# A long fused kernel on one core: x loaded once a batch and turned by VectorE instead of TensorE

## What is computed

```python
# 1: batch 4, heads 8, seq 768, head_dim 48
for t in range(S):
    state = alpha[:, :, t, :, None] * state + einsum('bhd,bhe->bhde', k[:, :, t], v[:, :, t])
    y[:, :, t] = einsum('bhd,bhde->bhe', q[:, :, t], state)
# 2: x is y with the heads side by side, (4, 768, 384)
theta = x @ w_theta
zr, zi = x * cos(theta), x * sin(theta)
y = einsum('ts,bsd->btd', w_tok_r, zr) + einsum('ts,bsd->btd', w_tok_i, zi)
u = x + y
x = u + maximum(u @ w_ch, 0)
# 3: d_ff 1024
h = maximum(x @ w_in, 0)
conv = sum over k of conv_w[k] * (h shifted by k - 1 tokens)
out = (h * sigmoid(conv)) @ w_out
```

## Time and profile before

| | us |
|---|---|
| three runs | 531.9, 532.3, 532.47 |
| median | 532.3 |
| span of the profiled execution, first to last instruction | 530.5 |
| TensorE busy in it | 522.1 |
| VectorE busy | 441.2 |
| ScalarE busy | 287.4 |

### The profile page before, as it was taken

How to read it: one execution, slowest core, us unless ns; L and a number is a source line. 1 busy time by engine, 2 the same in 40 slices (tenths; PEclk the granted TensorE clock), 3 DMA queues, 4 the chain that set the end, 5 groups by cost and what they waited for, 6 DMA issues and landing times.

```text
span 530.5 us, 11806 instructions
## 1 busy us (share of the span) xinstructions
PE 522.1 (98%) x4142; PEld 513.2 (97%) x4142; DVE 441.2 (83%) x801; ACT 287.4 (54%) x607; POOL 72.0 (14%) x65
## 2 busy tenths in 40 slices
PE   8999999999999999999999999999999999999997
PEld 7999988999999999999999999999999999999997
DVE  8999996997886759767786777999888888889874
ACT  4889887765534434444344542555555454545353
POOL 5988893000000000000000000000000000000000
PEclk9999999999999999999999999999999999999999
DMA  8999987476131020211062011202020110201011
GB/s 326 336 308 361 313 302 224 120 236 222 40 104 31 17 70 25 96 30 54 15 205 94 1 45 56 80 2 90 0 89 30 59 56 33 89 0 47 0 46 44
DMA packets 37163, 56.93 MB, mean 107 GB/s; under 512 B 3328, under 2 KB 27392, under 8 KB 37120
## 3 DMA queue, kind: packets, MB, share of 16 engines
q1 hardware_dynamic: 34000, 51.65, 29.3%
q10 hardware_dynamic: 3120, 4.72, 2.5%
HBM read 42.20 MB, written 14.16 MB: 106 GB/s over the span
## 4 chain that ended last, share of the span: by engine, by line
PE 92%; SPq 2%; DVE 2%; DMA 2%; issue 1%; ACT 0%; POOL 0%; DVEq 0%; ACTq 0%
PE y_bank L1475 26%; PE y_bank L1534 19%; PE theta_bank L1521 10%; PE x_bank L1521 10%; PE y_bank L1505 7%; PE theta_bank L1462 7%; PE weighed L1372 4%; PE x_sum L1330 3%; PE x_sum L1345 2%; PE turned L1357 2%; SPq L734 1%; PE x_bank L1450 1%; DMA x_in<-x_scratch 1%; PE turned L1377 1%; PE x_sum L1316 1%
## 5 line engine op out<-in xcount | busy, mean ns | idle before, releaser
L1534 PE MATMUL y_bank<-first_w,z 128*128 128x384 f32 x576 | 109.5, 335 | 0.0
L1534 PEld LDWEIGHTS y_bank<-first_w,z 128*128 128x128 f32 x576 | 101.2, 188 | 0.0
L1475 PE MATMUL y_bank<-first_w,z 128*128 128x384 f32 x432 | 78.0, 337 | 0.1
L1475 PE MATMUL y_bank<-rest_w,z 128*128 128x384 f32 x432 | 76.9, 336 | 0.0
L1475 PEld LDWEIGHTS y_bank<-first_w,z 128*128 128x128 f32 x432 | 74.5, 188 | 0.3 <-issue 0.3
L1475 PEld LDWEIGHTS y_bank<-rest_w,z 128*128 128x128 f32 x432 | 74.7, 188 | 0.0
L1045 ACT ACTIVATE out_rows<-theta_bank 128x386 f32<-128x386 f32 x32 | 15.8, 493 | 50.6 <-PE theta_bank L1521 50.5
L1275 DVE TENSOR_SCALAR x_rows<-out_rows,taps 128x384 f32<-128x384 f32 x64 | 26.8, 419 | 19.5 <-ACT out_rows L1045 19.4
L1462 PE MATMUL theta_bank<-theta_w,x_t 128*128 128x384 f32 x216 | 41.6, 336 | 0.1
L1278 DVE SCALAR_TENSOR_TENSOR x_rows<-out_rows,taps,x_rows 128x384 f32<-128x384 f32 x64 | 39.6, 619 | 2.3
L1282 DVE SCALAR_TENSOR_TENSOR z_full<-out_rows,taps,x_rows 128x384 f32<-128x384 f32 x64 | 39.6, 619 | 2.2
(11 more groups left out here) (126 smaller groups left out, 974.9 us busy)
## 6 DMA issues: line engine op xcount, KB each, us to landing
a_in<-in_a_rows SPq DMA_DIRECT2D x15, 390.0 KB, 5.8
k_in<-in_k_rows SPq DMA_DIRECT2D x15, 384.0 KB, 5.7
q_in<-in_q_rows SPq DMA_DIRECT2D x14, 384.0 KB, 5.3
v_in<-in_v_tokens SPq DMA_DIRECT2D x16, 288.0 KB, 4.8
x_in<-x_scratch SPq DMA_DIRECT2D x24, 192.0 KB, 2.5
y<-x_all SPq DMA_DIRECT2D x7, 576.0 KB, 3.2
u_scratch<-u_sum ACTq DMA_DIRECT2D x6, 576.0 KB, 3.5
u_first<-u_scratch SPq DMA_DIRECT2D x4, 577.5 KB, 4.4
```

What stands on the lines that cost most here:

```text
L1475: ins = pe.matmul(y_bank[2 * d + half][:, 0:HALF], z[s % 2][part][zp][:, d * P:(d + 1) * P], mixing_w(part, wp, s)[:, half_tokens(half)], ...
L1534: ins = pe.matmul(out_bank[half][t][:, 0:MODEL], g[k % 4][gp][:, t * P:(t + 1) * P], out_w[wp][f], start=f == 0 and i == 0, stop=f == FF_T ...
```

## The change

- Tiles of the mixing take other tokens: tile s takes tokens 32 s to 32 s + 31 of each quarter of 192 tokens. The token sums are over all tokens, so only the rows of the mixing weights are put into the same order, on the host in `laid_out`.
- x of a batch is loaded whole, 1152 KB in one DMA, into `x_even` or `x_odd`. `halve`, `lower` and the sums read it there. The tile loads, their three buffers and VectorE's copy into `x_all` go. Batch 0's load takes the place of the first tile load; batch b + 1 is loaded in step 2 of batch b.
- Four more DMAs a batch (`load_blocks`) load x again, quarter by quarter, into the partitions 0 to 31, 32 to 63, 64 to 95 and 96 to 127 of `x_blocks` (12 runs of 192 tokens on each partition). In batch 0 they follow the load of x; for batch b + 1 they are issued in step 4 of batch b, ahead of the loads of w_ch and of the w_in rows.
- `flip` (VectorE) turns 32 x 32 blocks of `x_blocks` into `x_tokens`, one instruction of 384 columns a tile. It stands ahead of the angles of the same tile. `turn` on TensorE and `hold` on ScalarE go.
- All four batches are written out; `y_out` lies in `x_even`; the scratch that the program reserves for another kind of DMA is made smaller.

```diff
@@ program, pair_step
             do.refill_piece(0)
             do.decide()
-            do.load_first(0)
+            do.load(0)
+            do.load_blocks(0)
             do.refill_piece(1)
-            do.load_first(1)
-            do.load_first(2)
@@ pair_tail
         do.store(o)
-        do.turn(0, 0)
         do.lower(0, 0)
         do.theta_low()
         do.theta(0, 0)
-        do.turn(0, 1)
         do.scan_state(p)
         do.low(0)
-        do.hold(0, 0)
+        do.flip(0, 0)
         do.high(1)
         do.halve(0, 1)
-        do.hold(0, 1)
         do.angle(0, 0)
@@ mix_batch
         for s in range(T):
-            tile(do.load, b, s + 3, last)
+            tile(do.flip, b, s + 1, last)
+            if s == T - 2 and not last:
+                do.load_blocks(b + 1)
             if s == T - 1:
                 do.mix(b, s)
                 do.sums(b)
             tile(do.halve, b, s + 2, last)
-            tile(do.hold, b, s + 2, last)
...
             tile(do.sines, b, s + 1, last)
-            tile(do.turn, b, s + 2, last)
             tile(do.lower, b, s + 2, last)
...
+            if s == 2 and not last:
+                do.load(b + 1)
@@
-    mix_batch(0)
-    with eng.Fori(1, LAST, 1) as b:
-        mix_batch(b)
-    mix_batch(LAST, True)
+    for b in range(BATCH):
+        mix_batch(b, b == LAST)
@@
+    def x_of(b, s):
+
+        return x_all[b % 2][:, :, :].rearrange("p a (g t) -> p a g t", g=GROUPS)[:, :, :, s * BLOCK:(s + 1) * BLOCK]
@@ sync
-        def load(b, s):
-            if isinstance(b, int) and b == 1 and s == 0:
+        def load(b):
...
+            if b == 1:
                 x_stored[0].done(sp, 2)
                 all_stored_late(sp, 0)
+                piece_low.done(sp, SPLIT_EARLY - 1)
+            if b == 2:
                 all_stored_late(sp, 1)
                 all_stored_late(sp, 2)
                 for u, t in enumerate(x_stored):
                     t.done(sp, stored_ahead(PAIRS + u))
+            if b >= 2:
+                u_done.done(sp, b - 2)
+            sp.dma_start(x_all[b % 2][:, :, :], x_scratch.rearrange("b (a p) t -> b p a t", p=P)[b, :, :, :]
+                         ).then_inc(x_got[b % 2].sem, 16)
+
+        def load_blocks(b):
+
+            if b:
+                x_flipped.done(sp, b * T - 1)
+            for g in range(GROUPS):
+                sp.dma_start(x_blocks[g * BLOCK:(g + 1) * BLOCK, :, :],
+                             x_scratch.rearrange("b (n p) (g t) -> b g p n t", p=BLOCK, g=GROUPS)[b, g, :, :, :]
+                             ).then_inc(blocks_got.sem, 16)
@@ scalar
         def halve(b, s):
             n = b * T + s
-            x_got[s % 3].done(act, b * (T // 3) + s // 3)
+            x_got[b % 2].done(act, b // 2)
             theta_made.before(act, n, 1)
             x_low.before(act, n, 1)
-            act.activation(x_t[0][:, :, :], x_in[s % 3][:, :, :], ACT.Copy).then_inc(x_high.sem, 1)
+            act.activation(grouped(x_t[0]), x_of(b, s), ACT.Copy).then_inc(x_high.sem, 1)
@@ vector
+        def flip(b, s):
+            n = b * T + s
+            blocks_got.done(dve, b)
+            z_done.before(dve, n, 2)
+            dve.transpose(x_tokens[s % 2][:, :].rearrange("p (n t) -> p n t", t=BLOCK), x_blocks[:, :, s * BLOCK:(s + 1) * BLOCK]
+                          ).then_inc(x_flipped.sem, 1)
@@ round_z
-            dve.tensor_copy(x_all[:, :, s * P:(s + 1) * P], x_in[s % 3][:, :, :]).then_inc(x_kept.sem, 1)
@@ tensor
-        def turn(b, s):
-            n = b * T + s
-            x_got[s % 3].done(pe, b * (T // 3) + s // 3)
-            x_moved.before(pe, n, 1)
-            if isinstance(b, int) and b == 0 and s == 0:
-                before_done.done(pe, LAST_PAIR)
-            for d in range(MODEL_TILES):
-                ins = pe.transpose(x_bank[:, d * P:(d + 1) * P], x_in[s % 3][:, d, :], ident[:, :])
-            ins.then_inc(x_turned.sem, 1)
@@ laid_out
-        out[x] = inputs[x].T
+        out[x] = inputs[x].T.reshape(GROUPS, TOKEN_TILES, BLOCK, SEQ).transpose(1, 0, 2, 3).reshape(SEQ, SEQ)
```

More of the change, by code:

```diff
@@ L223 @@
 PLACES = """refill_piece score scan_after scale_k spread cap by_token inside scan_before scale_q mask mask_late select added
-scan_state high bring keep low theta_high theta_low compare waves refill refill_v judge place divert decide store store_half store_late halve hold turn lower theta angle sines
-product round_z fill load load_first load_weight spare prepare mix sums end send join front gate split back_ff fetch""".split()
+scan_state high bring keep low theta_high theta_low compare waves refill refill_v judge place divert decide store store_half store_late halve flip lower theta angle sines
+product round_z fill load load_blocks load_weight spare prepare mix sums end send join front gate split back_ff fetch""".split()
 Work = namedtuple("Work", PLACES, defaults=[nothing] * len(PLACES))
@@ L352, in mix_batch @@
             tile(do.halve, b, s + 2, last)
-            tile(do.hold, b, s + 2, last)
-            if not (isinstance(b, int) and b == 0 and s == 0):
+            if not (b == 0 and s == 0):
                 tile(do.theta, b, s + 1, last)
@@ L367, in mix_batch @@
                 do.send(b, 0)
-            if isinstance(b, int) and b == 0:
+            if b == 0:
                 do.load_weight(s)
@@ L775, in spare @@
         def spare(b):
-            if isinstance(b, int):
-                all_stored_late(sp, 1)
-                all_stored_late(sp, 2)
-                for u, t in enumerate(x_stored):
-                    t.done(sp, stored_ahead(PAIRS + u))
             in_low.before(sp, b, 1)
@@ L835, in _ @@
         sp.sem_inc(c_got[0].sem, 16)
-        program(sp, Work(refill_piece=refill_piece, refill=refill, refill_v=refill_v, decide=decide, store=store, store_half=store_half, store_late=store_late, load_first=load_first,
-                         load=load, load_weight=load_weight, spare=spare, prepare=prepare, end=store_u, back_ff=back_ff))
+        program(sp, Work(refill_piece=refill_piece, refill=refill, refill_v=refill_v, decide=decide, store=store, store_half=store_half, store_late=store_late,
+                         load_blocks=load_blocks, load=load, load_weight=load_weight, spare=spare, prepare=prepare, end=store_u, back_ff=back_ff))
         stored[0].done(sp, BATCH - 1)
@@ L1127, in scan_before @@
             if i == 1:
-                for t in (x_low, turned_by, whole, first, second, bounded, z_done, x_kept, u_done, out_done,
+                for t in (x_low, turned_by, whole, first, second, bounded, z_done, u_done, out_done,
                           c_low, conv1_done, conv2_done, conv3_done, gated_done, z_low, g_low, in_low):
@@ L1227, in sums_of @@
         def sums_of(b):
[L1228 removed]
+            x_got[b % 2].done(dve, b // 2)
             for half in range(2):
@@ L1307, in _ @@
         program(dve, Work(scan_after=scan_after, scan_before=scan_before, place=place, mask=mask, scan_state=scan_state,
-                          divert=divert, lower=lower, angle=angles, fill=fill, product=product, theta_low=theta_low, low=low, round_z=round_z, load_weight=load_weight, sums=sums_of, end=end, spare=spare,
+                          divert=divert, lower=lower, flip=flip, angle=angles, fill=fill, product=product, theta_low=theta_low, low=low, round_z=round_z, load_weight=load_weight, sums=sums_of, end=end, spare=spare,
                           prepare=prepare, fetch=fetch, front=front, gate=gating, split=split))
@@ L1467, in mix @@
             n = b * T + s
-            first_batch = isinstance(b, int) and b == 0
+            first_batch = b == 0
             def add(half, part):
@@ L1510, in join @@
         def join():
-            x_moved.done(pe, LAST_TILE)
             first.done(pe, LAST_TILE)
```

64 lines of the change are left out of this document (29 added, 35 removed).

## The result

The changed kernel takes 534.7 us (median of five runs, 533.5 to 536.3) where the kernel before takes 532.3 (median of five, 531.3 to 532.5) on the same chip. The ratio is 1.0055, with a 95% interval of 1.0038 to 1.0072: slower by half a per cent. The forecast was 530.6. So its direction was wrong, and the time lies inside its range. The profiled execution spans 533.0 us, 2.5 more than before.

The account below looks back on a forecast made before the run. TensorE was taken to bound the kernel, busy 522.1 of 530.5 us. The terms -6.9 - 0.9 + 0.75 + 2.9 + 2.4 = -1.75, added to 532.3, gave 530.6 us, with a range of 527.2 to 535.0.

Parts of the forecast that it names:

- The turns, -6.9: Mixing steps: transposes leave TensorE's chain, 0.33 us a tile for 21 tiles, 6.9 us saved.
- The load wait, -0.9: Batch 0: a turn's 0.89 us wait for a tile of x queued behind stores goes.
- The covered wait, +0.75: Batch ends: without the turn TensorE waits for u before the channel product, some 0.25 us not gained, three times.
- The start, +2.9: Start of batch 0: the larger x load, the block loads and the flip make the angles 2.9 us later.
- One bound: Start of batch 0: at 273 GB/s, the lowest rate taken, the whole x load comes 3.8 us later.
- The end of batch 0, +2.4: End of batch 0: w_in rows queue behind the x and block loads, so the sums come 2.4 us late.
- The rest, 0: VectorE's copy replaced by the block transpose, ScalarE's copy gone, grouped reads, unrolled batches, permuted rows: no cost.
- all three rivals: Block loads at full rate (527.9, chance 0.22), at 205 to 174 GB/s (532.7, 0.25), or slower than before (535.2, 0.22).
- The third: Rival, slower than before: block loads at half of 333 GB/s, the rest at 333: +2.95, 535.2 us, chance 0.22.

Follow-up runs that it names:

- e7: The kernel before with every turn on TensorE made twice, six transposes a tile: 538.4 us, ratio 1.0117.
- e1: The changed kernel with idle 128-column matmuls in both TensorE gaps, 24 before the last pair's key products, 20 before batch 0's channel product: 533.95 us, ratio 1.0026.
- e4: The changed kernel with the next batch's block loads behind w_ch and the w_in rows, and its first flip behind the sums: 530.8 us, ratio 0.9971.
- e5: The changed kernel with the start reordered: theta behind two last-pair products, blocks behind the second weight piece, flip behind both: 535.3 us, ratio 1.005.
- e6: The changed kernel with the reordered start of e5 and the late block loads of e4 together: 531.4 us, ratio 0.9981.
- e10: The changed kernel with shorter idle matmuls of 64 columns in the two TensorE gaps, 14 and 12 of them: 533.4 us, ratio 1.0018.
- e11: e9 with the blocks loaded ahead of the second weight piece again and tile 1's low part ahead of the flip: 527.8 us, ratio 0.9927.
- e3: The changed kernel with ScalarE's high part of tile 0 moved behind the last pair's attention work: 533.9 us, ratio 1.0029.
- e2: The changed kernel with each block load filling all 128 partitions, same bytes and runs, output not the reference's: 531.1 us, ratio 0.998.
- e9: The changed kernel with e4's batch-end order and a second start order, tile 0's high part behind pair 14's x copies on ScalarE: 529.3 us, ratio 0.9942.
- e8: The same kernel as e1, run once more at another time: 535.6 us.

## Why the prediction was wrong

**1. The turns, -6.9: right.** The step went from 8.14 to 7.80 us, and e7 puts the reverse at +6.3.

**2. The load wait, -0.9: right.** Mixing and theta follow each other without a gap from 101.07 on.

**3. The covered wait, +0.75: too large.** In batches 1 and 2 the product starts as theta ends (206.34 + 1.56 = 207.90, start 207.91). What is lost there is only 0.15 and 0.20 us in the products themselves (9.54 and 9.57, where the chain before has 9.39 and 9.37). In batch 0 the wait is part of point 5.

**4. The start, +2.9: measured +5.3.** This is the step that failed. The load and the order were right: x landed in 5.8 us instead of 5.2, and everything up to the keys' product is 3.07 later instead of 2.7. The blocks moved at 212 to 221 GB/s, where I took 210, and the flip ended at 94.00 instead of 93.35: that is 0.65 of the miss. The other 1.8 is the clock. The angles did not start with the end of the flip, as I had it, but 1.76 us later, when theta was through, which took 3.25 us at half clock. At full clock, by the durations in e1's chain of waits, theta would have ended at 89.77 + 0.72 + 0.84 + 1.78 = 93.1, ahead of the flip, and part 4 would have been 94.00 - 90.43 = +3.6, an estimate. I had read that the clock was full "through all gaps of now", and priced its fall at nothing in the forecast and in no number of a rival. But TensorE's gaps in those rows were 0.40 and 0.89 us long, and there was none longer in that kernel once its first 8 us were over; the change made one of 3.7. (One bound does not come out of its own working: at 273 GB/s the fixed part is 2.5 - 0.197/0.273 = 1.8 us and the load is 3.6 later, not 3.8. Nothing hangs on it.)

**5. The end of batch 0, +2.4: the wait was nearly right, two waits of the queue and what follows the gap were missing.** Parts 3 and 5 together made the product wait 2.65 us; it waited 3.09. The w_in rows landed at 135.54 + 8.6 = 144.1, 3.3 after my 140.8. The load of x for batch 1 was issued at 125.31, 0.4 after my 124.9; but then I had let the queue run through, and it stood. Block loads overwrite the buffer of which the last flip still reads, and the waits of SP's queue say so:

```profile
SPq L783 <- DVE x_tokens L1195: 5.3, 1, 5.3
```

The flip of tile 5 ended at 133.1 and the four blocks were issued at 133.10. The stretch from 133 to 134 us shows 0 GB/s: what stood ahead had been moved, and the DMA engines had nothing to do. That wait is in VectorE's order, so the 2.4 us by which part 4 was short push it back too. w_ch has a wait of its own: it goes into a buffer that VectorE's split of a mixing weight frees, at 132.6 here, and in e4, where nothing stands before it, SP waits 4.2 us for that. So without the blocks' wait w_ch would not have gone 5.3 us earlier; what it loses is mainly the time in which the blocks, now ahead of it, are moved. Behind the gap the clock fell a second time: 11.21 us for the product instead of 9.54, 1.7 more, which the prediction put at nothing as well.

**6. The rest, 0: right.** The flip takes 0.57 us, the copy that it replaces 0.546.

With point 4 at +5.3, the wait at +3.1 and the second fall at +1.7: -6.9 - 0.9 + 0.3 + 5.3 + 3.1 + 1.7 = +2.6, against +2.5 measured. The two falls hold 1.8 + 1.7 = 3.5 of it. Without them the span would be 529.5 by this sum, not by a run, where the forecast had 528.8. The rest of the miss is the later landing at the start and the longer wait, less what part 3 had too much. The blocks' bandwidth, on which my range and all three rivals turned, was taken right, and none of the three came true. The third named the clock as something that might add to it, without a price and only there; it belonged into the forecast, or beside it as a rival with 3 to 4 us to it. That the time lies in the range is luck: it is owed to the room that the range kept for slow block loads.

**What stays open.** The fall does not follow on the length of a gap alone: 2.7 us in e5 and e6 was not enough, some microseconds behind an earlier fall, and in e10 1.6 us behind fillers of 64 columns was. What else decides it no run here tells. Nor do they tell why the slow stretch lasts 3.4 us in one execution and 6.8 in another. The two prices, 1.8 and 1.7 us, are read from the profiled execution; that the times of all executions differ by as much is not shown.

## What to carry to other kernels

Work taken from the engine that bounds is gained only where nothing else stops that engine: here 6.9 us were won in the steady steps and lost again at two seams. When a larger load takes the place of a small one, follow each engine's order behind it, and each wait of the queue that the change adds. Price a new gap of TensorE that is longer than those of the trace at hand as the gap plus, as a likely case, a stretch of half clock behind it (1.7 and 1.8 us here), less what a later wait would have cost anyway, and look first for an order that has no such gap: moving the blocks behind the loads that are wanted first was worth some 4 us here, and a new order at the start another 3 (e11 against e4).

## What the runs showed of the chip

**The clock.** Gaps of TensorE of 2.25 us (e11), 2.8 (e3, e5, e6), 3.1 and 3.7 (after), 3.3 (e2), 3.4 (e3, the later one), 3.5 (e4; e5, the last one) and 4.2 (e9) each went with half clock in the profiled execution, and so did one of 1.6 behind short fillers (e10). Gaps of 0.3 (e4), 0.4 and 0.9 (before), 1.2 (e3), 1.4 (e2; in the attention e5 and e8), 1.8 (before, among its first matmuls) and 2.7 (e5, e6, the later one) did not. The slow stretches last about 3.4 or 6.8 us. The executions of one kernel, by their mean clock:

| kernel | mean clock | spans, us |
|---|---|---|
| e9 | 1.0 | 525.3, 525.7 |
| e9 | 0.996 to 0.997 | 527.2 to 528.0 |
| e9 | 0.994 | 527.6, 529.3, 529.5 |
| after | 0.994 | 531.8, 532.2 |
| after | 0.990 | 533.0, 534.0, 534.6 |
| e1 | 0.999 to 1.0 | 531.8 to 532.5 |
| before, run beside e9 | 0.999 to 1.0 | 529.7 to 532.4 |

In e9 and after, a lower clock goes with a longer span. But the kernel before spreads over 2.7 us at full clock, and e8 shows 1.6 us lost in the attention alone. So how much of e9's 4 us is the clock these rows don't show.

**Few partitions.** In the kernel after, the stretches of 1 us that hold mainly loads into 32 partitions show 202 to 231 GB/s (88 to 92 and 136 to 140 us); those of e2, with the same run length into 128 partitions, show 328 to 363 (87 to 91). The Trainium skill, page "SBUF — State Buffer", section "Door 1: The DMA port swizzle", has 189 against 328 for 32 and 128 partitions at 1 MiB. The stretches here lie at or above these figures, and the ratio, about 0.6, agrees.

**The block transpose.** 24 of 128 x 384 took 571 ns each in the mean, 1.5 ns a column; the copy in the earlier trace rows has 1.4 (546 ns).
